# ScalarE's split instructions in front of an eviction at each block's end, and the first hidden tile in front of the last transposed phi products

## The reference

```python
attn_out = softmax(pooled(q) @ k.T / sqrt(D)) @ v        # 4 x 8 heads, 576 pooled queries, 1152 keys, D = 64
x = attn_out as 2304 tokens x 512
# mixture one: a Sinkhorn-weighted sum over 8 experts
P = exp(x @ w_gate - max);  8 rounds of row and column normalization
y = sum_e P[:, e] * (relu(x @ w1[e]) @ w2[e])            # w1[e] 512 x 1024, w2[e] 1024 x 512
# mixture two: soft slots, 32 of them
logits = y @ phi                                         # phi 512 x 32
d = softmax(logits, over tokens);  c = softmax(logits, over slots)
out = c @ expert_mlp(d.T @ y)                            # s_w1, s_w2
```

## Time and profile before

| what | value |
|---|---|
| median of 3 runs | 1754.67 us (1753.51 to 1755.44) |
| the profiled execution's own time | 1753.28 us |
| its span in the profile | 1751.5 us |
| mean granted clock of PE | 0.988 of full speed |
| PE busy | 1700.8 us, 97% of the span |
| DVE busy | 1024.3 us, 58% |
| ACT busy | 776.9 us, 44% |
| POOL busy | 418.8 us, 24% |
| largest group, line 1062, w_hi with x | 2304 products, 790.8 us |
| second, line 1062, w_lo with x | 1152 products, 449.9 us |

### The profile page before, as it was taken

The page is one execution under the profiler, slowest core; times in us unless marked ns, Lnnn a source line. Parts: engine busy times, 40 slices in busy tenths (PEclk is TensorE's granted clock), DMA queues, the critical chain, the costliest instruction groups (busy, mean ns, idle before and its releaser), DMA issues.

```text
span 1751.5 us, 31771 instructions
## 1 busy us (share of the span) xinstructions
PE 1700.8 (97%) x13225; PEld 1305.2 (75%) x13225; DVE 1024.3 (58%) x1306; ACT 776.9 (44%) x1161; POOL 418.8 (24%) x319
## 2 busy tenths in 40 slices
PE   7999999999999999999999999999999999999975
PEld 6888888888876877777777777777777777777434
DVE  6888787878754555555555555555555555555201
ACT  3444444444466444444444444454444444444101
POOL 3788888888810000000000000000000000000000
PEclk9999999999999999999999999999999999999997
DMA  9531322322035444443443444444434434454998
GB/s 300 144 82 42 79 45 65 59 46 52 15 133 193 157 151 141 142 144 133 145 145 132 155 135 141 137 141 136 145 133 146 147 131 153 156 192 167 386 420 337
DMA packets 159390, 258.57 MB, mean 148 GB/s; under 512 B 46784, under 2 KB 65216, under 8 KB 153536
## 3 DMA queue, kind: packets, MB, share of 16 engines
q1 hardware_dynamic: 159248, 256.54, 44.7%
HBM read 251.79 MB, written 9.96 MB: 149 GB/s over the span
## 4 chain that ended last, share of the span: by engine, by line
PE 63%; DMA 3%; DVE 2%; ACT 2%; issue 1%; SPq 0%; DVEq 0%
PE ring L1062 44%; PE ring L1072 7%; PE ring L1084 4%; PE ring L1119 4%; DMA wring<-in_moe_w_dram 2%; DMA xraw<-in_moe_w_dram 1%; PE ring L974 1%; DVE w_lo L1350 1%; PE ring L985 1%; ACT w_hi L1248 1%; PE ring L1170 1%; PE ring L1190 1%; ACT x_split L1240 0%; PE ring L1095 0%; ACT hring L1255 0%
## 5 line engine op out<-in xcount | busy, mean ns | idle before, releaser
L1062 PE MATMUL ring<-w_hi,x_split 128*128 128x512 f32 x2304 | 790.8, 404 | 3.3 <-DVE w_lo L1350 2.5
L1062 PEld LDWEIGHTS ring<-w_hi,x_split 128*128 128x128 f32 x2304 | 432.8, 188 | 116.7 <-issue 24.6
L1062 PE MATMUL ring<-w_lo,x_split 128*128 128x512 f32 x1152 | 449.9, 391 | 0.0
L1350 DVE TENSOR_TENSOR w_lo<-w_raw,w_hi 128x1024 fp32r<-128x1024 f32 x288 | 356.6, 1239 | 155.5 <-ACT w_hi L1248 155.5
L1293 ACT ACTIVATE wring<-ring,pw 128x512 f32<-128x512 f32 x218 | 150.1, 689 | 435.5 <-PE ring L1062 435.5
L1392 DVE COPY h_t<-ring 128x512 f32<-128x512 f32 x288 | 199.1, 691 | 236.6 <-PE ring L1072 236.5
L584 POOL TENSOR_TENSOR acc<-acc,pt 128x576 f32<-128x576 f32 x210 | 297.5, 1417 | 28.1
L1248 ACT ACTIVATE w_hi<-w_raw 128x1024 fp32r<-128x1024 f32 x288 | 302.6, 1051 | 0.0
L1528 POOL TENSOR_TENSOR x_split<-xraw,x_split 128x512 fp32r<-128x512 f32 (+1 forms) x20 | 23.6, 1185 | 980.0 <-ACT x_split L1240 980.0
L515 DVE TENSOR_REDUCE neg_part<-ring 116x2 f32<-116x768 f32 (+1 forms) x240 | 228.8, 958 | 43.7 <-PE ring L303 24.4
L1062 PEld LDWEIGHTS ring<-w_lo,x_split 128*128 128x128 f32 x1152 | 217.5, 189 | 37.9
(11 more groups left out here) (212 smaller groups left out, 1692.8 us busy)
## 6 DMA issues: line engine op xcount, KB each, us to landing
w_raw<-in_moe_w_dram SPq DMA_DIRECT2D x288, 512.0 KB, 3.5
wring<-in_moe_w_dram SPq DMA_DIRECT2D x34, 1024.0 KB, 10.0
q_raw<-in_q_dram SPq DMA_DIRECT2D x32, 288.0 KB, 5.9
v_raw<-in_v_dram SPq DMA_DIRECT2D x16, 576.0 KB, 4.5
xraw<-in_moe_w_dram SPq DMA_DIRECT2D x9, 1024.0 KB, 14.7
k_raw<-in_k_dram SPq DMA_DIRECT2D x30, 288.0 KB, 7.1
hring<-in_moe_w_dram SPq DMA_DIRECT2D x6, 1024.0 KB, 21.1
out_dram<-wring SPq DMA_DIRECT2D x8, 512.0 KB, 6.1
```

Source lines behind the costliest of these rows:

```text
L1062: last = pe.matmul(h_ps[n % 3][:, :], a[:, k, toks], w[:, k, :], start=(k == 0 and m == 0), stop=(k == DK - 1 and m == 2))
L1350: dve.tensor_tensor(w1_lo[v % 2][:, 2 * c:2 * c + 2, :], w1_raw[:, 2 * (p % RAWS):2 * (p % RAWS) + 2, :], w1_hi[v % 2][:, 2 * c:2 * c + 2, ...
```

## The change

Two edits. In the phi stage `turn_phi(2)` and `keep_phi(2)` move from behind slice 56 to behind slice 63, the last (so ahead of `times_phi(3)` on PE and of `keep_wp(3)` on ACT), and `turn_phi(3)` on PE moves behind `hidden(0)`; ACT's order of `keep_wp(3)`, `keep_phi(3)`, `keep(0)` stays. In the hidden tiles, at the last unit's first tile of blocks 0 to 7, ACT does `split_x` and `split_w1` ahead of `keep(n)` rather than behind it. DVE's, POOL's and SP's programs are the same.

```diff
@@ PE, phi stage @@
-                if i % 16 == 8 and i > 16:
+                if i % 16 == 8 and 16 < i < STEPS - 16 + 8:
                     turn_phi(i // 16 - 1)
+            turn_phi(QUADS - 2)
             times_phi(QUADS - 1, (0, 1, 2, 3))
-            turn_phi(QUADS - 1)
@@ PE, hidden tiles @@
             for n in range(TILES):
                 hidden(n)
+                if n == 0:
+                    turn_phi(QUADS - 1)
                 if n >= 1:
                     turn(n - 1)
@@ ACT, phi stage @@
-                if i % 16 == 8 and i > 16:
+                if i % 16 == 8 and 16 < i < DK * UNITS - 16 + 8:
                     keep_phi(i // 16 - 1)
+            keep_phi(QUADS - 2)
             keep_wp(QUADS - 1)
             keep_phi(QUADS - 1)
@@ ACT, hidden tiles @@
+                urgent = u == UNITS - 1 and i == 0 and b + 1 < NB
+                if urgent:
+                    split_x(b + 1, 0)
+                    split_w1(PIECES * (v + 1) + 1)
                 keep(n)
-                if u == UNITS - 1 and b + 1 < NB:
+                if u == UNITS - 1 and b + 1 < NB and not urgent:
                     split_x(b + 1, i)
...
-                if i == 0 and v + 1 < UNITS * NB:
+                if i == 0 and v + 1 < UNITS * NB and not urgent:
                     split_w1(PIECES * (v + 1) + 1)
```

## The result

The changed kernel's median is 1749.84 us over 11 runs, beside 1754.98 us for the kernel before on the same chip: a ratio of 0.9967, 95% interval 0.9952 to 0.9981. The forecast was 1751.0, 3.7 us won. One of the eleven executions of the changed kernel took 7888.61 us and is left out of the ratio; without it the median is 1749.82 us.

A forecast was written before the change was run, and what follows sets the result against it. PE was taken to bound the kernel, carrying 63% of the chain, so only its standing still could be won. Block ends 3.0 plus start 0.65 gave 3.7 us, a median of 1751.0, range 1749.2 to 1754.0.

The forecast's parts named there:

- The block ends: At eight block ends PE's waits for w_lo go: 7 x 0.35 + 0.57 = 3.0 us won.
- The start: At the first hidden tiles, hidden(2) starts at 564.95 instead of 565.60: 0.65 us won.
- The new wait in front of hidden(2): At the start, PE waits 0.5 us for w_lo, behind ACT's keep_phi(3), eviction and weight split.
- rival E: At block ends, the eviction queues behind a split waiting for late weights: 11.4 us lost, 1766; chance 0.04.
- rival B: At block ends, DVE's PSUM copy locks the port, delaying POOL and w_lo: almost only the start wins, 1753.9; chance 0.12.
- the other meeting, POOL against w_lo: At block ends, POOL's last 0.40 us lie over w_lo; their offset stays, so w_lo's 1.48 us stays.
- rival D: In the ending, the weight stream is bound by something that does not move: no gain, 1754.7; chance 0.06.
- the last step: From profiled execution to median: 1753.28 us, 1.4 below the runs' median, would become 1749.6; the median then becomes 1751.0.
- A's better bound: A is the forecast, block ends and start: 3.7 us won (3.2 to 4.3), 1751.0; own range 1749.8 to 1752.2; chance 0.70.

The follow-up runs named there:

- c_xonly: Changed kernel, but at a block's end only the token split goes ahead of the eviction, the weight split behind it: 1751.72 us, ratio 0.9986 against the kernel before.
- a_before: The kernel before with no edit, run again against itself: 1754.61 us, ratio 1.0002.
- a_ends: The kernel before with only the edit at the block ends: 1750.63 us, ratio 0.9980 against the kernel before.
- a_after: The changed kernel with both edits, run a second time: 1750.33 us, ratio 0.9977 against the kernel before.
- b_inner: Changed kernel with ACT's weight split moved ahead of the exponential at a block's third step: 1748.20 us, ratio 0.9966 against the kernel before.
- c_wonly: Changed kernel, but at a block's end only the weight split goes ahead of the eviction, the token split behind it: 1751.41 us, ratio 0.9984 against the kernel before.

## Why the prediction was right or wrong

**Which waits go, and by how much.** Right in mechanism and place, a little low in size. The block ends were put at 3.0 and gave 3.3 us: I had summed the tags of the weight loads, 0.35, where the distance between successive transposes shows 0.37 and 0.57, 3.2 in all; the last 0.1 is within what H repeats. The start was put at 0.65 and gave 0.8: hidden(0) begins 10.48 us after ACT's copy before and 8.81 after the change, 1.67 earlier where I had 1.53. The 0.14 between them is all that was missed, for hidden(2) was put at 564.95, 15.90 after the copy, and came at 15.76. The new wait in front of hidden(2), put at 0.5, is 0.50.

**The eviction behind the split, rival E.** It ends 0.63 us ahead of the transposes, where 0.53 was worked out; no weight piece came late.

**The port, rival B.** POOL and DVE's copy out of PSUM keep their 1.30 and 0.69 us with 0.42 of overlap. What I did not see is that the other meeting, POOL against w_lo, was a term of the wait itself: 0.25 of the 1.48, which c_xonly takes away. I carried it over as "stays", which held for this change only because both moved by the same 0.59.

**The ending, rival D.** It moves with the hidden tiles. T lies between 104.9 and 106.2 in 14 profiles whatever the edit, and the longest five, 105.9 to 106.2, are those with the longer half clock after the last tile.

**What was wrong is the last step**, the level and the spread, and not a wait: "with the same step the median becomes 1751.0", and below it "A's better bound with the spread of a median, 1749.2". The step took the median of three runs, 1754.67, as the level from which to count, and left 1.8 us beneath the forecast for a larger gain and for the spread together. That was too little: the first comparison drew 2.0 us more than the 3.8 that all the runs together show. The executions of the kernel before fall into two groups, whose times overlap at the edges. In the 83 runs of the three later comparisons, 30 have a mean granted clock under 0.9895 and a median of 1755.02 us, 53 have more and 1753.68; the median of all is 1753.86. The changed kernel's 32 runs, all but the one of 7888.61 us, split into 9 with 1750.52 and 23 with 1749.79, in all 1750.07. The changed kernel was 1749.84, 1750.33 and 1749.96 in its three comparisons; it is the kernel before that was at 1754.98 in the first and at 1753.8 to 1753.9 after. That a draw of eleven can do this is shown by a_before: the same program, 8 of 11 executions with the lower mean clock, 1754.61. Over all of these runs the gain is 1753.86 - 1750.07 = 3.8 us, and within a group 3.9 to 4.5. The first comparison's ratio, 0.9967, put on 1754.67, is 1748.9 and lies under the range; that is 5.8 won, 2.0 more than the 3.8. The same comparison's medians give 5.1, and 1749.5, within the range. The ratio's interval reaches 0.9981 and holds the 0.9977 of the other two. So the draw was bad luck, and the error is to have left no more room for it.

What the profiles show is where the groups part. The five with a mean clock of 0.987 or 0.988 (before, a_before, a_ends, a_after, b_inner) are the five with the longest T, 106.0 on average; the nine others, at 0.990 to 0.993, have 105.25. So some 0.8 us of the distance between the groups, 1.3 in the kernel before and 0.7 in the changed one, lies behind the last tile. What stays open is why an execution falls into one group or the other, and why the first comparison drew the slower one more often; that it did is read from its times, for its executions of the kernel before have no clock on record. In the profiles the lower clock comes between 35 and 45 us in some, between 510 and 520 in others and in one in both, and this does not go with the groups; the edits do not sort it either.

## What to carry to other kernels

Where PE waits for a chain over several engines, look on each engine of the chain for what stands ahead of the wanted instruction in program order and is wanted later; an eviction with 0.6 us of slack, or an exponential that itself waits, can go behind it. Then look at what runs beside each link: part of its time may be a wait for another engine, as 0.25 us of w_lo's 1.48 were here. Sum by the distance between repeated instructions rather than by tagged waits, compare executions over stretches with a common first instruction, and take the level of a kernel from more than three runs when its executions come in groups.

## What the runs showed of the hardware

DVE's subtraction with both inputs in SBUF and POOL's subtraction hold each other up, and the order of their starts says who pays. POOL first (905.98 to 907.28): w_lo, started at 906.88, ends 1.08 us after POOL. DVE first (905.88 to 907.10 in c_wonly): POOL, started at 906.11, ends 1.13 us after DVE. The first one keeps its own time in both cases, 1.30 and 1.22. It is the same at every meeting: in the kernel before, w_lo ends 1.08 us after POOL all 16 times, also at 788 us, where the overlap is 0.53 us and w_lo takes 1.61. The Trainium skill (SBUF — State Buffer, "Who interferes with whom") calls it an exclusive lock in which whoever issues first makes the other block fully. The trace agrees as to who pays; the second ends 0.15 us sooner than a whole instruction after the first (1.08 for 1.23, 1.13 for 1.30), as if its first 0.15 us were not held up. By that the 0.25 us for 0.40 of overlap, which the prediction read as less than full blocking, is full blocking less that 0.15. The same section's exemption for a VectorE instruction with at most one input in SBUF, outside the two-port modes, agrees too: the copy out of PSUM took 0.69 us and POOL 1.30 with 0.42 us of overlap.
